# The rows of x turned by VectorE and moved through memory, in a two-layer mixture-of-experts kernel

## The chip, the cores and the metric

The kernel runs on one core of a Trainium2 chip. The metric is the device time of one execution in microseconds (us), the median of three runs. TensorE multiplies, VectorE and ScalarE work on what it leaves, GpSimd issues the indirect DMAs (rows picked by an index), SyncE the loads of weights. All DMAs run on 16 shared DMA engines.

## What is computed

```python
x = attention(q, k, v, mem_k, mem_v)              # (3072, 512) after a reshape
# layer 1: each row of x goes to its best 2 of 8 experts
logits = x @ w_gate + np.log1p(np.exp(x @ w_noise)) * noise
for e in range(8):
    for k in range(2):
        mask = top2[:, k] == e
        h = np.maximum(x[mask] @ w1[e], 0.0)      # (rows, 512) @ (512, 1024)
        out[mask] += top2_w[mask, k, None] * (h @ w2[e])
# layer 2: the same on that output, the best 1 of 8, other weights
        out[mask] = gate_w[mask, None] * (np.maximum(xe @ w1[e], 0.0) @ w2[e])
```

All in float32. The kernel keeps float32 precision by splitting each operand in a high and a low part and adding three products (high by high, high by low, low by high).

## The kernel before

A front part computes attention, gates and routing tables (to about 190 us, and a second, shorter one from about 766 to 860 us). The rest is the two expert layers, class `Experts`, instances `x` and `z`. Rows are sorted by expert and cut in tiles of 128, each with one expert: 53 tiles in the first layer, 27 in the second. What is said here of tile t holds for both.

For one tile: GpSimd copies the row numbers to `from_row` and gathers 128 rows of x (`gather`, L1552) into `xg`. TensorE turns them by four transposes of 128x128 (`x_transposes`, L1594) into PSUM `ps_x`, since a product wants the 512 inputs on the partitions. ScalarE writes the high part `x_hi` (`high_x`, L1672), VectorE the low part `x_lo` (`low_x`, L1699). `first_product` is 24 matmuls of 512 columns into `ps_h`. h is not turned by TensorE: VectorE turns it in blocks of 32x32 in two instructions (`turn`, L1710) into `h_turned`, ScalarE's queue stores that to the memory tensor `h_d` (`park`, L1658) and reads it back in four DMAs with the blocks in their places (`fetch`, L1667) into `h_moved`. There is one `h_d` and one `h_moved`: a park waits until the fetch before it has landed (semaphore `moved`), and a fetch waits until `low_h` has read the last contents (`h_split`). ScalarE makes `h_hi` (`high_h`, L1681), VectorE `h_lo` in four instructions (`low_h`, L1719). `second_product` is 24 matmuls into `ps_y`; ScalarE weighs the result by its gate into `y` (`weigh`, L1693), and GpSimd adds it to the output rows (`scatter`, L1580; in the second layer it stores them, L1583).

The order is written out by hand in one loop for each engine, and each engine works through its own in order. TensorE (`tensor_loop`), iteration t: first product t+1, transposes t+2, second product t-1. ScalarE (`scalar_loop`): high_x t+2, park t+1, high_h t, weigh t-1, fetch t+1. VectorE (`vector_loop`): some pieces of the next expert's weights (`splits`, L141 and L147, two instructions each), turn t+1, low_x t+2, more pieces, low_h t. How many pieces stand at the two places of a tile is in two tables (`before`, `middle`) that the kernel works out from the routing. GpSimd (`pool_loop`): wait for the transposes t+3, keep the gate t+3 (`keep_gate`, L1561, copies one column of `xg`), gather t+4, scatter t. Below, a tile of VectorE is called light when no pieces stand between low_x and low_h, and heavy when two do. A period is the time from one tile's transposes to the next tile's.

## Time and profile before

| | us |
|---|---|
| median of three runs | 1152.98 (1149.24 to 1154.13) |
| the profiled execution, its own time | 1158.04 |
| its span in the trace | 1156.1 |
| TensorE busy | 1094.8 |
| VectorE busy | 643.2 |
| GpSimd busy | 317.6 |
| ScalarE busy | 279.9 |

Busy time is the time in which an engine executed something; a share is of the span. The mean granted clock of TensorE in the profiled execution was 0.963 of 2.4 GHz. In a timeline, the bracket at a row's end gives how long the engine had been idle before it, and what ended the wait. A row of a queue (ACTq) is the issue of a DMA, not its transfer.

### The profile page before, as it was taken

To read this page: it belongs to the slowest core of one execution; us is meant where nothing else is said; L and a number is where in the kernel's file an instruction comes from. 1 tells how busy PE (TensorE), PEld (TensorE's weight loads), DVE (VectorE), ACT (ScalarE), POOL (GpSimd) and SP (SyncE) were. 2 spreads that over 40 slices of the span, in tenths; PEclk is the share of its full clock that TensorE was granted. 3 is DMA by queue.
4 is the path that set the end of the run, shared out by engine and by line. 5 is a ranking of instruction groups with operands and counts; after the bars stand their busy time and mean duration, and the time that the engine had idled before them with its cause. 6 is when DMAs were issued, how large, how long until landed. Compare 5 with 4: busy or idle time off the path is not lost. (4 is left out here: it accounts for less than half of the span.)

```text
span 1156.1 us, 29685 instructions
## 1 busy us (share of the span) xinstructions
PE 1094.8 (95%) x7939; PEld 886.5 (77%) x7940; DVE 643.2 (56%) x1360; ACT 279.9 (24%) x534; POOL 317.6 (27%) x474
## 2 busy tenths in 40 slices
PE   5989888999999999999999999979989999999997
PEld 4767766888888888888888888856567888877785
DVE  2767586655553552644635436306876336666862
ACT  3566321121211212121212112115212121212121
...
GB/s 344 348 344 280 294 273 148 239 221 217 183 234 143 213 209 137 227 196 165 235 175 204 219 135 211 137 96 270 61 246 241 193 124 219 247 232 236 303 222 88
DMA packets 126990, 245.87 MB, mean 213 GB/s; under 512 B 17454, under 2 KB 70878, under 8 KB 126960
## 3 DMA queue, kind: packets, MB, share of 16 engines
...
q10 hardware_dynamic: 61728, 90.25, 24.2%
...
q8 instruction: 14, 0.23, 0.1%
...
## 5 line engine op out<-in xcount | busy, mean ns | idle before, releaser
L1601 PE MATMUL moe_ps_h<-weights,moe_x_hi 128*128 (+1 forms) x640 | 253.8, 397 | 11.2 <-ACT moe_x_hi L1672 7.9
L1601 PE MATMUL moe_ps_y<-weights,moe_h_hi 128*128 (+1 forms) x624 | 251.6, 403 | 6.4 <-ACT moe_h_hi L1681 4.9
L1602 PE MATMUL moe_ps_h<-weights,moe_x_hi 128*128 (+1 forms) x640 | 251.8, 393 | 0.0
L1602 PE MATMUL moe_ps_y<-weights,moe_h_hi 128*128 (+1 forms) x624 | 244.5, 392 | 0.0
L1719 DVE SCALAR_TENSOR_TENSOR moe_h_lo<-moe_h_moved,moe_h_hi 128x256 fp32r<-128x256 f32 x312 | 111.5, 420 | 228.6 <-ACT moe_h_hi L1681 228.6
L1606 PE MATMUL moe_ps_h<-weights,moe_x_lo 128*128 (+1 forms) x640 | 172.9, 392 | 0.0
L1681 ACT ACTIVATE moe_h_hi<-moe_h_moved 128x1024 fp32r<-128x1024 f32 x78 | 82.7, 1060 | 371.0 <-PE moe_ps_y L1606 301.6
L147 DVE TENSOR_TENSOR weights<-stage,weights (+1 forms) x128 | 156.7, 1225 | 19.7 <-DVE weights L141 19.7
L1606 PE MATMUL moe_ps_y<-weights,moe_h_lo 128*128 (+1 forms) x624 | 154.1, 389 | 0.0
L1601 PEld LDWEIGHTS moe_ps_h<-weights,moe_x_hi 128*128 128x128 f32 x640 | 121.6, 190 | 41.5 <-issue 13.8
L1601 PEld LDWEIGHTS moe_ps_y<-weights,moe_h_hi 128*128 128x128 f32 x624 | 117.9, 189 | 31.5 <-issue 6.1
L1606 PEld LDWEIGHTS moe_ps_h<-weights,moe_x_lo 128*128 128x128 f32 x640 | 121.5, 190 | 25.6
L1602 PEld LDWEIGHTS moe_ps_h<-weights,moe_x_hi 128*128 128x128 f32 x640 | 121.7, 190 | 25.2 <-issue 0.2
L1672 ACT ACTIVATE moe_x_hi<-moe_ps_x 128x512 fp32r<-128x512 f32 x82 | 49.1, 599 | 374.1 <-PE moe_ps_x L1594 289.3
L1710 DVE STREAM_TRANSPOSE moe_h_turned<-moe_ps_h 128x512 f32<-128x512 f32 x160 | 107.5, 699 | 57.6 <-issue 35.7
L1606 PEld LDWEIGHTS moe_ps_y<-weights,moe_h_lo 128*128 128x128 f32 x624 | 117.1, 188 | 24.3
L1602 PEld LDWEIGHTS moe_ps_y<-weights,moe_h_hi 128*128 128x128 f32 x624 | 118.0, 189 | 22.4
L1580 POOL DMA_INDIRECT x_d<-moe_y,moe_to_row x51 | 82.7, 1621 | 187.0 <-ACT moe_y L1693 185.1
L141 DVE TENSOR_SCALAR weights<-stage (+1 forms) x124 | 85.1, 687 | 74.8 <-issue 74.7
L1552 POOL DMA_INDIRECT moe_xg<-x_d,moe_from_row x83 | 99.5, 1199 | 72.0 <-POOL moe_from_row L1546 35.4
L1561 POOL COPY routes_gate<-moe_xg (+2 forms) x81 | 17.7, 218 | 202.7 <-PE moe_ps_x L1594 194.4
L1699 DVE TENSOR_TENSOR moe_x_lo<-moe_ps_x,moe_x_hi 128x512 fp32r<-128x512 f32 x82 | 55.0, 671 | 26.0 <-ACT moe_x_hi L1672 26.0
...
## 6 DMA issues: line engine op xcount, KB each, us to landing
stage<-in_w SPq DMA_DIRECT2D x128, 512.0 KB, 4.5
...
moe_h_moved<-h_d ACTq DMA_DIRECT2D x320, 128.0 KB, 3.4
...
```

The costliest lines, as they stand in the source:

```text
L141: dve.tensor_scalar(weights[:, to, :], stage[:, frm, :], 1.0, None, ALU.mult).then_inc(sem("w_high"), 1)
L147: dve.tensor_tensor(weights[:, to + NCHUNK, :], stage[:, frm, :], weights[:, to, :].bitcast(F32), ALU.subtract).then_inc(sem("split"), 1)
L1552: pool.indirect_dma_start(xg[:, :], None, self.x_rows[0:among, :], at, bounds_check=among - 1, oob_is_err=True).then_inc(s("gathered_b" if ...
L1580: d = pool.indirect_dma_start(self.y_rows, at, y[:, :], None, bounds_check=NPAD - 1, oob_is_err=True, compute_op=ALU.add)
L1601: pe.matmul(out, a_hi, b_hi, start=(i == 0), stop=False)
L1602: pe.matmul(out, a_hi, b_lo, start=False, stop=False)
L1606: mm = pe.matmul(out, a_lo, b_hi, start=False, stop=(i == len(parts) - 1))
L1672: act.activation(self.x_hi[:, :, :], self.ps_x[:, :, :], ACT.Copy).then_inc(self.s("x_high"), 1)
L1681: act.activation((self.h_hi_end if end else self.h_hi)[:, :, :].rearrange("p c (a q) -> p c a q", a=QB), self.h_moved[:, :, :, :].rearrang ...
L1699: dve.tensor_tensor(self.x_lo[:, :, :], self.ps_x[:, :, :], self.x_hi[:, :, :].bitcast(F32), ALU.subtract)\
L1710: dve.transpose(self.h_turned[:, 2 * f:2 * f + 2, :, :].rearrange("p b c q -> p (b c q)"), self.ps_h[:, f, :]).then_inc(s("turned"), 1)
L1719: last = dve.scalar_tensor_tensor(out=h_lo[:, :, cols], in0=self.h_moved[:, a, :, :], scalar=0.0, in1=h_hi[:, :, cols].bitcast(F32), op0=A ...
```

## The change

In the loops of both layers TensorE turns no rows of x any more. From tile 5 in the first layer and tile 4 in the second, VectorE turns them in blocks of 32x32 in one instruction (`turn_x`) into a new buffer `x_turned`. ScalarE's queue stores it to a new memory tensor `xt_d` (`park_x`) and reads it back in four DMAs (`fetch_x`) into a new buffer `x_moved`, in contiguous runs of 128 numbers (h: 256). `high_x` and `low_x` read `x_moved` in SBUF instead of `ps_x` in PSUM; `high_x` then waits for the first product before it by a semaphore of its own, since no transposes stand between. The semaphores are `x_parked` and `x_moved`; `xt_done` is now counted up by turn_x. The first tiles still go over TensorE.

The order changes with it. VectorE, tile t: pieces, turn t+1, low_x t+2, **turn_x t+4**, pieces, low_h t. ScalarE: high_x t+2, park t+1, **fetch_x t+3**, high_h t, weigh t-1, fetch t+1, **park_x t+4**. GpSimd: **scatter t first**, then wait for tile t+5 to be turned, keep its gate, **gather t+6** (LAG = 5). So scatter t and gather t+6 fall in the same period, and VectorE turns that row tile in the next one. At the start of each layer one more tile is gathered ahead into a second buffer `xg_b`. The number of pieces at each place, the weight loads and all products are as before.

```diff
+LAG = 5
...
             x.gather(pool, 0)
-            for t in range(1, EARLY):
-                pool.wait_ge(s("xt_done"), t)
-                x.keep_gate(pool, t - 1)
-                x.gather(pool, t)
+            x.gather(pool, 1, second=True)
+            pool.wait_ge(s("xt_done"), 1)
+            x.keep_gate(pool, 0)
+            x.gather(pool, 2)
+            pool.wait_ge(s("xt_done"), 2)
+            x.keep_gate(pool, 1, second=True)
...
             x.scatter(pool, 0)
-            m = x.tiles(pool)
-            pool.wait_ge(s("xt_done"), EARLY + 1)
-            x.keep_gate(pool, EARLY)
-            x.gather(pool, EARLY + 1)
-            x.pool_loop(pool, 1, m)
+            m = x.gathered_ahead(pool)
+            pool.wait_ge(s("xt_done"), 4)
+            x.keep_gate(pool, 3)
+            x.gather(pool, 4)
+            x.gather(pool, 5, second=True)
+            pool.wait_ge(s("xt_done"), 5)
+            x.keep_gate(pool, 4)
+            x.gather(pool, 6)
+            pool.wait_ge(s("xt_done"), 6)
+            x.keep_gate(pool, 5, second=True)
+            pool.memset(x.xg_b[:, DM:DM + E], 0.0)
+            x.pool_loop(pool, m)
...
-        self.gathers = 16 if routes.k == 2 else 0
+        self.turned_from = 5 if routes.k == 2 else 4
+        self.xt_d = xt_d
+        self.x_blocks = xt_d.rearrange("(a p) (b r) -> b p a r", a=QB, b=QB)
...
+            self.x_turned = sb("x_turned", [P, QB, DC, QR])
+            self.x_moved = sb("x_moved", [P, QB, DC, QR])
...
+    def gathered_ahead(self, eng):
+        return self.table(eng, self.routes.full, 1, self.routes.least + 1 - LAG, self.routes.tiles + 1 - LAG)
...
+    def park_x(self, act, t):
+        s, n = self.s, t - self.turned_from
+        act.wait_ge(s("xt_done"), t + 1)
+        if not (isinstance(t, int) and n == 0):
+            act.wait_ge(s("x_moved"), n * (16 * QB))
+        act.dma_start(self.xt_d, self.x_turned[:, :, :, :].rearrange("p b c q -> p (b c q)"))\
+           .then_inc(s("x_parked"), 16)
+    def fetch_x(self, act, t):
+        s, n = self.s, t - self.turned_from
+        act.wait_ge(s("x_parked"), n * 16 + 16)
+        act.wait_ge(s("x_split"), t)
+        for b in range(QB):
+            act.dma_start(self.x_moved[b * QR:(b + 1) * QR, :, :, :].rearrange("p a c q -> p a (c q)"),
+                          self.x_blocks[b]).then_inc(s("x_moved"), 16)
+    def high_x(self, act, t, moved=False):
+        s, n = self.s, t - self.turned_from
+        if moved:
+            act.wait_ge(s("x_moved"), n * (16 * QB) + 16 * QB)
+            act.wait_ge(s("l1_done"), t * 2)
+            act.nop(nofuse=True)
+            act.activation(self.x_hi[:, :, :].rearrange("p c (a q) -> p c a q", a=QB),
+                           self.x_moved[:, :, :, :].rearrange("p a c q -> p c a q"), ACT.Copy).then_inc(s("x_high"), 1)
+        else:
+            act.wait_ge(s("xt_done"), t + 1)
+            act.activation(self.x_hi[:, :, :], self.ps_x[:, :, :], ACT.Copy).then_inc(s("x_high"), 1)
...
-    def low_x(self, dve, t):
+    def low_x(self, dve, t, moved=False):
         dve.wait_ge(self.s("x_high"), t + 1)
-        dve.tensor_tensor(self.x_lo[:, :, :], self.ps_x[:, :, :], self.x_hi[:, :, :].bitcast(F32), ALU.subtract)\
-           .then_inc(self.s("x_split"), 1)
+        if moved:
+            last = dve.tensor_tensor(self.x_lo[:, :, :].rearrange("p c (a q) -> p c a q", a=QB),
+                                     self.x_moved[:, :, :, :].rearrange("p a c q -> p c a q"),
+                                     self.x_hi[:, :, :].bitcast(F32).rearrange("p c (a q) -> p c a q", a=QB),
+                                     ALU.subtract)
+        else:
+            last = dve.tensor_tensor(self.x_lo[:, :, :], self.ps_x[:, :, :], self.x_hi[:, :, :].bitcast(F32),
+                                     ALU.subtract)
+        last.then_inc(self.s("x_split"), 1)
+    def turn_x(self, dve, t, second=False):
+        s, xg = self.s, self.xg_b if second else self.xg
+        if second:
+            dve.wait_ge(s("gathered_b"), 32)
+        else:
+            dve.wait_ge(s("gathered"), t * 16 - 16)
+            dve.wait_ge(s("x_parked"), (t - self.turned_from) * 16)
+        dve.nop(nofuse=True)
+        dve.transpose(self.x_turned[:, :, :, :].rearrange("p b c q -> p c b q"),
+                      xg[:, 0:DM].rearrange("p (c b q) -> p c b q", c=DC, b=QB)).then_inc(s("xt_done"), 1)
...
-        def tile(t, end=False):
+        def tile(t, first=False, end=False):
             frm, mid, to = self.counts(dve, t, (before, t), (middle, t), (before, t + 1))
             dve.wait_ge(s("l2_done"), t)
             dve.nop(nofuse=True)
             self.splits(dve, frm, mid)
             self.turn(dve, t + 1)
-            self.low_x(dve, t + 2)
+            if not end:
+                self.low_x(dve, t + 2, moved=not first)
+            if first:
+                self.turn_x(dve, t + 3, second=True)
+            if not first and not end:
+                self.turn_x(dve, t + 4)
             self.splits(dve, mid, to)
             self.low_h(dve, t, end)
-        with dve.Fori(begin, m) as t:
+            if first:
+                self.turn_x(dve, t + 4)
+        tile(begin, first=True)
+        with dve.Fori(begin + 1, m) as t:
             tile(t)
         tile(m, end=True)
...
     def scalar_loop(self, act, begin, m):
-        def tile(t, end=False):
-            self.high_x(act, t + 2)
+        def tile(t, first=False, end=False):
+            if not end:
+                self.high_x(act, t + 2, moved=not first)
             self.park(act, t + 1)
+            if first:
+                self.park_x(act, t + 3)
+            elif not end:
+                self.fetch_x(act, t + 3)
             self.high_h(act, t, end=end)
             if end:
                 self.fetch(act, t + 1)
...
             else:
                 self.weigh(act, t - 1)
                 self.fetch(act, t + 1)
-        with act.Fori(begin, m) as t:
+            if first:
+                self.fetch_x(act, t + 3)
+            if not end:
+                self.park_x(act, t + 4)
+        tile(begin, first=True)
+        with act.Fori(begin + 1, m) as t:
             tile(t)
         tile(m, end=True)
         self.high_h(act, m + 1, last=m)
         self.weigh(act, m, end=True)
         self.weigh(act, m + 1, last=True)
+        near = self.gathered_ahead(act)
+        act.wait_ge(self.s("x_parked"), near * 16 + (3 - begin) * 16)
+        act.wait_ge(self.s("x_moved"), near * (16 * QB) + (2 - begin) * (16 * QB))
+        act.nop(nofuse=True)
     def tensor_loop(self, pe, begin, m):
         with pe.Fori(begin, m + 1) as t:
             self.first_product(pe, t + 1)
-            self.x_transposes(pe, t + 2)
             self.second_product(pe, t - 1)
         self.second_product(pe, m, end=True)
         self.second_product(pe, m + 1, last=True)
-    def pool_loop(self, pool, begin, m):
+    def pool_loop(self, pool, m):
         s = self.s
-        with pool.Fori(begin, m) as t:
-            pool.wait_ge(s("xt_done"), t + 4)
+        with pool.Fori(1, m) as t:
+            self.scatter(pool, t)
+            pool.wait_ge(s("xt_done"), t + (LAG + 1))
             pool.nop(nofuse=True)
-            self.keep_gate(pool, t + 3)
-            self.gather(pool, t + 4)
-            self.scatter(pool, t)
-        self.scatter(pool, m, end=True)
-        self.scatter(pool, m + 1, last=True)
-        pool.wait_ge(s("gathered"), m * 16 + (48 + self.gathers))
+            self.keep_gate(pool, t + LAG)
+            self.gather(pool, t + (LAG + 1))
+        for i in range(LAG - 1):
+            self.scatter(pool, m + i, end=(i == LAG - 3), last=(i == LAG - 2))
+        pool.wait_ge(s("gathered"), m * 16 + (LAG - 1) * 16)
         if self.add:
-            pool.wait_ge(s("scattered"), m * 16 + 32)
+            pool.wait_ge(s("scattered"), m * 16 + (LAG - 1) * 16)
         else:
-            pool.wait_ge(s("scattered"), m * 16 + 16)
+            pool.wait_ge(s("scattered"), m * 16 + (LAG - 2) * 16)
             pool.wait_ge(s("scattered_last"), 16)
         pool.nop(nofuse=True)
...
+        xt_d = nc.dram_tensor("xt_d", [P, DM], F32, kind="Internal").ap()
```

VectorE, in the loop of the first layer, from the second turn of h to the wait of the pieces behind low_x. Before (`ps_h` is the first product; `staged` is the loaded piece of weights):

```order
L1710 STREAM_TRANSPOSE moe_h_turned<-moe_ps_h 128x512 [waits moe1_l1_done]
L1698 REGISTER_ALU
L1699 TENSOR_TENSOR moe_x_lo<-moe_ps_x,moe_x_hi 128x512 [waits moe1_x_high]
L1725 COMPARE_AND_BRANCH
L1726 UNCONDITIONAL_BRANCH
L1726 ISA
L141 REGISTER_ALU [waits staged]
```

With the change:

```order
L1783 STREAM_TRANSPOSE moe_h_turned<-moe_ps_h 128x512 [waits moe1_l1_done]
L1752 REGISTER_ALU
L1754 TENSOR_TENSOR moe_x_lo<-moe_x_moved,moe_x_hi 128x512 [waits moe1_x_high]
L1769 ISA
L1770 ISA [waits moe1_gathered]
L1772 STREAM_TRANSPOSE moe_x_turned<-moe_xg 128x4x4x32 [waits moe1_x_parked]
L1798 COMPARE_AND_BRANCH
L1799 UNCONDITIONAL_BRANCH
L1799 ISA
L142 REGISTER_ALU [waits staged]
```

The row with `moe_x_turned` has moved in between low_x and the pieces, with a wait for `gathered` and one for `x_parked`.

ScalarE, in the same loop, from its second step on. Before:

```order
L1655 ISA
L1657 REGISTER_ALU [waits moe1_turned]
L1658 DMA h_d<-moe_h_turned 128x1024 [waits moe1_moved]
L1679 ISA [waits moe1_l2_done]
L1681 ACTIVATE moe_h_hi<-moe_h_moved 128x1024 [waits moe1_moved]
L1693 ISA [waits moe1_gated,moe1_l2_done,moe1_y_free]
L1693 ACTIVATE moe_y<-moe_ps_y,routes_gate 128x512
L1663 ISA
L1667 DMA moe_h_moved<-h_d 32x4x256 [waits moe1_h_split,moe1_parked]
```

With the change:

```order
L1681 ISA
L1683 REGISTER_ALU [waits moe1_turned]
L1684 DMA h_d<-moe_h_turned 128x1024 [waits moe1_moved]
L1708 ISA
L1709 REGISTER_ALU [waits moe1_x_parked]
L1711 DMA moe_x_moved<-xt_d 32x4x128 [waits moe1_x_split]
L1711 DMA moe_x_moved<-xt_d 32x4x128 x3
L1732 ISA [waits moe1_l2_done]
L1734 ACTIVATE moe_h_hi<-moe_h_moved 128x1024 [waits moe1_moved]
L1746 ISA [waits moe1_gated,moe1_l2_done,moe1_y_free]
L1746 ACTIVATE moe_y<-moe_ps_y,routes_gate 128x512
```

The four DMAs `moe_x_moved<-xt_d` have moved in between the park of h and high_h; the fetch of h (L1693) and the store of x (L1702) follow.

GpSimd, in the same loop, from the loop's head. Before, it begins with the gate:

```order
L1561 ISA
L1561 COPY routes_gate<-moe_xg 128x1
L1481 ISA [waits moe1_gated]
L1481 TENSOR_LOAD routes_place
L1481 ISA x2
L1546 ISA
L1546 COPY moe_from_row<-routes_row 128x1
L1548 REGISTER_ALU
L1552 DMA moe_xg<-x_d,moe_from_row 128x520 [waits moe1_from_row]
```

With the change it begins with the scatter, and the gate's copy and the gather come behind:

```order
L1598 COPY moe_to_row<-routes_row 128x1
L1600 REGISTER_ALU
L1601 REGISTER_ALU [waits moe1_to_row]
L1605 DMA x_d<-moe_y,moe_to_row 3200x520 [waits moe1_y_ready]
L1893 REGISTER_ALU
L1503 ISA [waits moe1_xt_done]
L1503 TENSOR_LOAD routes_expert
L1503 ISA x2
L1586 ISA
L1586 COPY routes_gate<-moe_xg 128x1
```

The scatter, which waits for y, now stands ahead of the gather.

## Rows read from the trace of the kernel before

**Rows 1.** The page: busy us (share of span) and count; queue: packets, MB, share.
```profile
PE 1094.8 (95%) x7939; PEld 886.5 (77%) x7940; DVE 643.2 (56%) x1360; ACT 279.9 (24%) x534; POOL 317.6 (27%) x474
...
q10 hardware_dynamic: 61728, 90.25, 24.2%
```

**Rows 2.** Stretches: length, busy time of each engine, clock, DMA share, GB/s.
```profile
430.22:441.57 11.35, 11.35 (x54) 9.40 (x52) 3.55 (x7) 2.24 (x3) 3.26 (x5) 1.00 0.53 139
464.27:475.62 11.35, 11.35 (x54) 9.40 (x52) 8.80 (x13) 2.24 (x3) 3.67 (x5) 1.00 0.92 269
1058.00:1107.00 49.00, 46.55 (x210) 37.44 (x209) 41.84 (x60) 8.95 (x12) 20.32 (x21) 1.00 0.89 282
```

**Rows 3.** Transposes of x in each layer's loop: count, ns min/median/max, first and last start.
```profile
L1594 PE MATMUL moe_ps_x<-ident,moe_xg x192: 270/272/273, 214.6 to 748.3; 128*128 128x128 f32 x192
...
L1594 PE MATMUL moe_ps_x<-ident,moe_xg x96: 270/272/273, 862.2 to 1130.4; 128*128 128x128 f32 x96
```

**Rows 4.** Timeline of TensorE around one tile's transposes: start, duration.
```profile
407.52 0.60 PE L1594 MATMUL moe_ps_x<-ident,moe_xg 128*128 128x128 f32 x4
407.87 0.48 PE L1601 MATMUL moe_ps_y<-weights,moe_h_hi 128*128 x1
408.19 0.39 PE L1602 MATMUL moe_ps_y<-weights,moe_h_hi 128*128 x1
408.42 0.40 PE L1601 MATMUL moe_ps_y<-weights,moe_h_hi 128*128 x1
```

**Rows 5.** Timeline of ScalarE and its queue in a light tile.
```profile
427.74 1.76 ACTq L1667 DMA_DIRECT2D moe_h_moved<-h_d  x4
...
433.79 0.34 ACTq L1658 DMA_DIRECT2D h_d<-moe_h_turned  x1
436.47 1.06 ACT L1681 ACTIVATE moe_h_hi<-moe_h_moved 128x1024 fp32r<-128x1024 f32 x1 [5.01 <-PE moe_ps_y L1606]
437.43 0.67 ACT L1693 ACTIVATE moe_y<-moe_ps_y,routes_gate 128x512 f32<-128x512 f32 x1
439.07 1.76 ACTq L1667 DMA_DIRECT2D moe_h_moved<-h_d  x4
```

**Rows 6.** Timeline of GpSimd in the same tile and the next.
```profile
438.97 1.61 POOL L1580 DMA_INDIRECT x_d<-moe_y,moe_to_row  x1 [4.02 <-ACT moe_y L1693]
443.03 0.18 POOL L1561 COPY routes_gate<-moe_xg  x1 [2.46 <-PE moe_ps_x L1594]
...
445.02 1.08 POOL L1552 DMA_INDIRECT moe_xg<-x_d,moe_from_row  x1 [0.83 <-DMA x_d<-moe_y,moe_to_row]
```

**Rows 7.** Timeline of VectorE: a light tile, then a heavy one.
```profile
430.49 0.72 DVE L1710 STREAM_TRANSPOSE moe_h_turned<-moe_ps_h 128x512 f32<-128x512 f32 x1 [0.60 <-PE moe_ps_h L1606]
...
437.56 1.43 DVE L1719 SCALAR_TENSOR_TENSOR moe_h_lo<-moe_h_moved,moe_h_hi 128x256 fp32r<-128x256 f32 x4 [5.38 <-ACT moe_h_hi L1681]
...
463.49 0.69 DVE L141 TENSOR_SCALAR weights<-stage  x1 [1.80 <-issue]
464.36 1.23 DVE L147 TENSOR_TENSOR weights<-stage,weights  x1 [0.17 <-DVE weights L141]
465.50 1.30 DVE L1710 STREAM_TRANSPOSE moe_h_turned<-moe_ps_h 128x512 f32<-128x512 f32 x2
466.73 0.65 DVE L1699 TENSOR_TENSOR moe_x_lo<-moe_ps_x,moe_x_hi 128x512 fp32r<-128x512 f32 x1
467.31 0.67 DVE L141 TENSOR_SCALAR weights<-stage  x1
...
471.61 1.43 DVE L1719 SCALAR_TENSOR_TENSOR moe_h_lo<-moe_h_moved,moe_h_hi 128x256 fp32r<-128x256 f32 x4 [0.24 <-ACT moe_h_hi L1681]
```

**Rows 8.** DMA issues (KB, us to landing), and the indirect ones of both layers.
```profile
moe_h_moved<-h_d ACTq DMA_DIRECT2D x320, 128.0 KB, 3.4
...
L1552 POOL DMA_INDIRECT moe_xg<-x_d,moe_from_row x83: 1032/1080/2044, 137.0 to 1132.9; - x83
...
DMA to landing us min/median/max: 3.3/4.5/7.5
...
L1583 POOL DMA_INDIRECT out<-moe_y,moe_to_row x25: 1023/1032/2014, 860.2 to 1142.2; - x25
```

**Rows 9.** Timelines in the second layer: GpSimd beside two pieces; VectorE's low_h, consecutive heavy tiles.
```profile
1062.51 2.03 POOL L1552 DMA_INDIRECT moe_xg<-x_d,moe_from_row  x1 [0.85 <-POOL moe_from_row L1546]
...
1069.32 1.42 DVE L1719 SCALAR_TENSOR_TENSOR moe_h_lo<-moe_h_moved,moe_h_hi 128x256 fp32r<-128x256 f32 x4
...
1081.53 1.42 DVE L1719 SCALAR_TENSOR_TENSOR moe_h_lo<-moe_h_moved,moe_h_hi 128x256 fp32r<-128x256 f32 x4
```

**Rows 10.** Pieces of weights split in the loop of each layer: count.
```profile
L141 DVE TENSOR_SCALAR weights<-stage x56: 669/691/696, 236.8 to 724.6; - x56
...
L141 DVE TENSOR_SCALAR weights<-stage x48: 670/686/714, 863.5 to 1126.3; - x48
```

**Rows 11.** Timeline of TensorE: the third tile's transposes.
```profile
162.23 0.94 PE L1594 MATMUL moe_ps_x<-ident,moe_xg 128*128 128x128 f32 x4 [2.01 <-DMA moe_xg<-x_d,moe_from_row]
```

33 lines of the change are left out of this document (19 added, 14 removed).

## The prediction

> **What bounds the kernel now.** I read the summary first: TensorE 95% busy, VectorE 56%, ScalarE 24% [rows 1]. The share of an average says little, so next the table of stretches. A light tile of the first expert layer (no weights to split) takes 11.35 us, with TensorE full and the clock at 1.00, that is 2.4 GHz; so does a heavy one, with VectorE busy 8.80 us and the DMA engines at 0.92; in the second layer a run of heavy tiles has TensorE idle for 2.45 of 49 us at a DMA share of 0.89 [rows 2]. The count of transposes gives the whole: 192, four to a tile, from 214.6 to 748.3 us, so 47 periods of 11.35 us = 533.4 us in the first layer; 96 from 862.2 to 1130.4 us, so 23 periods = 267.8 us in the second (11.64 us each) [rows 3]. So TensorE bounds the first layer outright. The other engines run in step, and what they have is slack inside a period, not time to give away. The question is which slack the change uses up.
>
> **What is removed.** Transposes begin at 407.52 and the second matmul behind them at 408.19; matmuls follow each other by 0.23, so the four cost TensorE 0.67 - 0.23 = 0.44 us [rows 4]. Take 0.45: a period that TensorE bounds falls from 11.35 to 10.90 us. 73 of the 82 groups go, 49 and 24. If nothing else came late that would be 73 x 0.45 = 33 us. VectorE's subtraction reads SBUF in place of PSUM: 0.65 us before, against half of the 1.23 of one 1024 wide from SBUF, 0.62 [rows 7], so nothing.
>
> **What is added on ScalarE, and where it lies.** ScalarE's loop through h is a closed chain: fetch of h issued at 427.74, all of it landed and so h_d free and the next park issued at 433.79 (6.05 us); high_h starts at 436.47, held only by TensorE; it takes 1.06, VectorE's low_h 1.43 follows, and the next fetch is issued at 439.07, 2.60 us after high_h began [rows 5]. Without TensorE's hold this chain would take 6.05 + 0.34 + 2.60 = 9.0 us of 11.35. The change puts the four issues of the x fetch between park and high_h. Four issues of the same kind hold the queue for 1.76 us [rows 5]. Chain: 6.05 + 0.34 + 1.76 + about 0.1 to hand over + 2.60 = **10.85 us**, against the new period of 10.90. A light tile thus still fits, with nothing left; a delay, once there, is no longer made up. The store of x and its issue come behind the fetch of h, off this chain.
>
> **What is added on VectorE, and what it waits for.** One transpose of 128x512 per tile, from SBUF: 0.65 us by its sibling from PSUM (1.30 for two); bounds 0.35, half of the split's first operation of 0.69 on 1024 columns in SBUF, and 0.72, a sibling that stands alone [rows 7]. What matters is its place: behind low_x and ahead of the second splits and of low_h, and behind a wait for the gather. GpSimd now scatters a tile before it gathers the one that VectorE turns in the next tile. From high_h's end at 437.53 [rows 5]: scatter starts 1.44 later at 438.97 and takes 1.61; from the gate copy to the gather's start is 445.02 - 443.03 = 1.99 [rows 6]; between scatter and gate copy I take 0.4 (the rows allow 0, as the copy behind the gather starts at once, to 0.9, the wait of the others); issue to landing is 4.5 us, 3.3 to 7.5 [rows 8]. The row of x is there 1.44 + 1.61 + 0.4 + 1.99 + 4.5 = 9.94 us after high_h's end, and turned at 10.6. The next low_h may start at 10.9. So in a light tile the wait is covered by VectorE's idle time ahead of low_h, 5.38 us in such tiles [rows 7].
>
> In a **heavy tile** it is not covered. Before, the two splits of the second half ran from 467.31 and low_h followed at 471.61, 4.3 us later and only 0.24 of it a wait [rows 7]: they began as soon as low_x was done. Now they begin when the gather has come. 9.94 + 0.65 + 0.3 (branch and loop no longer hidden behind a queued operation; 0 to 0.5) + 4.0 = **14.9 us** from high_h's end to the next low_h, against 10.85. Behind low_h stand the fetch of h on ScalarE, hence the park, the x fetch, high_h and the weighing, and then TensorE's second product. A heavy tile delays the chain by 4.0 us.
>
> **Where the Trainium skill is weighed against the trace.** Beside VectorE's splits a gather's issue on GpSimd takes 2.03 us [rows 9], by the median 1.08 [rows 8], 0.95 more. The gather now comes 12 to 13 us after the end of a first product, where the next tile's first split may run; 14.9 + 0.95 = 15.8 us is the upper value of a heavy tile, and I take the median row since of two heavy tiles in four the split may miss it. The Trainium skill states this as a rule (SBUF — State Buffer, the box on the "DVE blocks DMA" trap: a DMA of GpSimd's queue waits for its descriptors while VectorE holds the shared port pair in a two-port operation). The skill has a rule against the change itself (VectorE: DVE Perf Modes, Rules for kernel authors): a 128x128 transpose belongs on TensorE where PSUM will do as the destination. By the rule the loss would be there in every tile; by the rows the two cost 0.44 us of one engine and 0.65 of the other, and only the waits decide.
>
> **The sum.** First layer: 56 pieces are split in the loop [rows 10], eight for each of seven experts, in four tiles as 3, 1, 3, 1, so 14 heavy tiles of the 47. 14 x 14.9 + 33 x 10.9 = 568.3; less the slack before TensorE is reached, once. high_h's results are wanted when the second product starts, 0.35 behind 441.57; the weighing ends at 438.10, so 3.8, and 3.5 with the shorter period [rows 2, 5]. 564.8 against 533.4: **+31**. Second layer: 48 pieces, four to a tile, so 12 heavy tiles [rows 10], 7 of them behind a light one. Its scatter takes 1.03 in place of 1.61 [rows 8], so 14.3 each; the 5 that follow a heavy tile are bound by VectorE itself, 12.21 from one low_h to the next [rows 9], plus 0.65 and 0.3 = 13.2; 11 light ones at 10.9. 100.1 + 66.0 + 119.9 - 3.5 = 282.5 against 267.8: **+15**. Startup: the third tile waited 2.01 us for its gather [rows 11], which is now issued a tile earlier: **-2**, or nothing if the routing tables end the wait instead. DMA: the queue of h moved 90.25 MB in 24.2% of the span, 280 us, so 3.1 us a MB [rows 1]; x's round trip is 0.52 MB a tile, 1.6 us of all engines. Its store is issued right behind the fetch of h, whose landing is in the chain. Bounds: 0, and 1.6 in each of the 44 light tiles, 70 us. I take 0.35, under half of the store's 0.8: **+15**. Together 31 + 15 - 2 + 15 = **+59**. The profiled execution took 1158.0 us (span 1156.1 and 1.9 around it), 5 above the median of 1153.0. 1217 on its scale, 1212 on the median's, of which I give **1210**.
>
> **Rivals.** The floor of all of them is 70 periods of 10.9 us, 763 against the 801.2 of before, so -38. (1) *The waits are shorter than I give them, and the kernel gains.* h's fetch lands in 5.5 us (one issue of it lands in 3.4 [rows 8], and the fourth is issued 1.4 behind the first), so a light tile makes up 0.6; the gather lands in its least of 3.3, and the 0.4 and 0.3 fall away, so a heavy tile takes 1.44 + 1.61 + 1.99 + 3.3 + 0.65 + 4.0 = 13.0, 2.1 over the period. 26 x 2.1 = 55, less 44 x 0.6 = 26 made up, less the slack of 3.5 twice: +22. With -38 and -2: 1158 - 18 = 1140, 1135 on the median's scale. With no loss at all 1118. For it: light tiles are not late by my sum either, and the losses are sums of guesses of a few tenths. Against: nothing in the order takes the second splits from behind the wait. (2) *The DMA engines become the bound.* Share 0.92 of 11.35 is 10.4 us in a heavy tile [rows 2]; with 1.6 more it is 12.0, over the period, and each landing in the chain grows. 0.5 us more in each of the 44 light tiles (+22) and 15.8 for a heavy one (26 x 0.9 = +23): 1255. (3) *A wash.* As (1), but a heavy tile 2.9 over: 26 x 2.9 = 75, less 26 and 7, less 40: +2, that is 1155. That the change doesn't do what it says is left out: the order has no transposes of x in TensorE's loops; the five and four tiles ahead of them are in the sum.
>
> **How the numbers follow.** The forecast (the chain closes at about 10.9 us and heavy tiles stretch it) 0.60; the DMA bound 0.17; the gain 0.17; the wash 0.06. The point is the forecast's, 1210. Its own range is 1175 to 1240. The wide one reaches into both outer cases and leaves out the far half of the gain and the top of the DMA case: 1130 to 1262. A measurement of this kernel tells about 0.5%, 6 us, from no change. Faster by more than that (below 1147): 0.17; within it: 0.06; slower: 0.77.
>
> **What would show it.** Right: no transposes of x on TensorE in the loops, and light tiles at 10.9 to 11.4 us; the new transpose on VectorE idle in front of it, released by the gather; in heavy tiles low_h late and TensorE waiting for high_h, for y or for the turned h, three or four us each; ScalarE's high_h released by DMA or by VectorE, no longer by TensorE. Wrong: TensorE full through the first layer with periods of 10.9 (then the chain is shorter than I add it up: the first suspect is the 6.05 us, the second the gather's place), or heavy tiles no longer than light ones, or gathers that land before low_x is done.

## The result: slower by an eighth, in the direction forecast and outside its range

| | before | with the change |
|---|---|---|
| median, us | 1153.56 (1149.24 to 1155.27) | 1300.78 (1292.16 to 1307.11) |
| ratio | | 1.124, 95% interval 1.119 to 1.130 |
| profiled execution: span, us | 1156.1 | 1296.8 |
| TensorE: busy, us; granted clock of 2.4 GHz | 1094.8; 0.963 | 1114.1; 0.941 |

The forecast was 1210 with a range up to 1262. The page of the changed kernel, the lines that answer to [rows 1], then the groups of its fifth section with idle time (count | busy us, mean ns of one | idle us before it, and what ended most of that):

```profile
PE 1114.1 (86%) x7647; PEld 872.7 (67%) x7648; DVE 695.5 (54%) x1435; ACT 281.1 (22%) x532; POOL 327.9 (25%) x475
...
q10 hardware_dynamic: 114576, 129.07, 31.8%
...
L1627 PE MATMUL moe_ps_h<-weights,moe_x_hi 128*128 (+1 forms) x640 | 271.2, 424 | 98.0 <-DVE moe_h_turned L1783 70.8
L1627 PE MATMUL moe_ps_y<-weights,moe_h_hi 128*128 (+1 forms) x624 | 252.5, 405 | 29.0 <-ACT moe_y L1746 23.0
...
L1734 ACT ACTIVATE moe_h_hi<-moe_h_moved 128x1024 fp32r<-128x1024 f32 x78 | 82.7, 1060 | 457.9 <-issue 428.9
...
L1772 DVE STREAM_TRANSPOSE moe_x_turned<-moe_xg 128x512 f32<-128x512 f32 x73 | 51.9, 712 | 203.2 <-DMA moe_xg<-x_d,moe_from_row 158.5
```

TensorE is busy for 19 us more, though it does less, and idle in front of both products: 98 us before the first product, mostly for VectorE's turn of h, 29 us before the second, mostly for ScalarE's weighing. VectorE's new transpose has 203 us of idle time ahead of it, 158 until a gather lands and 45 until the store of the x before has landed. The 429 us of `high_h` are put down to nothing: it waits on semaphores that the page can't place, so its wait is read from the timeline.

Stretches, with the columns of [rows 2]: a light tile (from one first product to the next), a heavy one (from one high_h to the next), a second product behind idle time, and 49 us of light tiles of the second layer.

```profile
577.31:588.75 11.44, 11.20 (x50) 8.96 (x49) 4.15 (x8) 2.27 (x3) 3.65 (x5) 1.00 0.70 185
430.25:447.06 16.81, 13.37 (x57) 10.07 (x55) 9.73 (x15) 2.26 (x3) 3.93 (x5) 1.00 0.80 223
449.16:456.35 7.19, 7.19 (x25) 5.81 (x26) 4.14 (x7) 0.63 (x1) 3.70 (x5) 0.76 0.77 197
1015.00:1064.00 49.00, 49.00 (x218) 40.57 (x217) 18.75 (x37) 10.71 (x14) 11.86 (x22) 1.00 0.61 194
```

From high_h to high_h the 32 light tiles of the first layer's loop take 11.8 us on average, with TensorE not full, and the 15 heavy ones 16.8. In the second layer a run of light tiles has TensorE full at 10.88 us a tile. The clock is 0.76 on average in the third stretch. TensorE's timeline there:

```profile
440.96 0.49 PE L1627 MATMUL moe_ps_h<-weights,moe_x_hi 128*128 x1 [2.86 <-DVE moe_h_turned L1783]
...
449.16 0.49 PE L1627 MATMUL moe_ps_y<-weights,moe_h_hi 128*128 x1 [2.47 <-ACT moe_y L1746]
...
450.39 0.63 PE L1627 MATMUL moe_ps_y<-weights,moe_h_hi 128*128 x1
450.82 0.63 PE L1628 MATMUL moe_ps_y<-weights,moe_h_hi 128*128 x1
...
453.37 0.39 PE L1628 MATMUL moe_ps_y<-weights,moe_h_hi 128*128 x1
453.60 0.39 PE L1627 MATMUL moe_ps_y<-weights,moe_h_hi 128*128 x1
```

TensorE was idle for 2.86 us ahead of one product and 2.47 ahead of the next, and in that one the matmuls stand 0.43 us apart for 3.4 us (1.2 GHz), in place of 0.23 (2.4 GHz). The product takes 7.19 us in place of 5.44.

**Where the time went**, by the starts of TensorE's phases in both traces. Up to the transposes of the fourth tile: 184.09 us in place of 186.74, -2.7. From there to the last second product in the first layer's loop (two more follow behind it), 663.1 in place of 561.6: +101.4. From that to the first transpose of the second layer 75.8 in place of 71.6: +4.1. From that transpose to the last second product in the second layer's loop 348.3 in place of 310.4: +37.9. Behind that the two are equal. The sum is the +140.7 between the spans. The forecast had +31 and +15 for the layers and +15 for the DMA engines.

ScalarE in a light tile, the answer to [rows 5]:

```profile
583.66 1.76 ACTq L1693 DMA_DIRECT2D moe_h_moved<-h_d  x4
585.61 0.34 ACTq L1702 DMA_DIRECT2D xt_d<-moe_x_turned  x1
586.45 0.63 ACT L1721 ACTIVATE moe_x_hi<-moe_x_moved 128x512 fp32r<-128x512 f32 x1 [3.76 <-issue]
589.67 0.34 ACTq L1684 DMA_DIRECT2D h_d<-moe_h_turned  x1
590.40 2.20 ACTq L1711 DMA_DIRECT2D moe_x_moved<-xt_d  x4
592.78 1.06 ACT L1734 ACTIVATE moe_h_hi<-moe_h_moved 128x1024 fp32r<-128x1024 f32 x1 [5.70 <-issue]
...
595.39 1.76 ACTq L1693 DMA_DIRECT2D moe_h_moved<-h_d  x4
```

From fetch to fetch: 6.01 (583.66 to 589.67) + 0.34 + 0.39 + 2.20 + 0.18 + 2.61 = **11.73 us**; forecast were 6.05 + 0.34 + 1.76 + 0.1 + 2.60 = 10.85. The next park waits for nothing but the landing.

A heavy tile: GpSimd, VectorE and ScalarE, the answers to [rows 6, 7]. The high_h ahead of the scatter began at 418.18.

```profile
420.68 1.61 POOL L1605 DMA_INDIRECT x_d<-moe_y,moe_to_row  x1 [4.62 <-ACT moe_y L1746]
...
424.29 1.49 POOL L1577 DMA_INDIRECT moe_xg<-x_d,moe_from_row  x1 [0.82 <-POOL moe_from_row L1571]
```

```profile
429.75 0.71 DVE L1772 STREAM_TRANSPOSE moe_x_turned<-moe_xg 128x512 f32<-128x512 f32 x1 [3.13 <-DMA moe_xg<-x_d,moe_from_row]
430.53 0.69 DVE L142 TENSOR_SCALAR weights<-stage  x1
...
434.53 1.42 DVE L1792 SCALAR_TENSOR_TENSOR moe_h_lo<-moe_h_moved,moe_h_hi 128x256 fp32r<-128x256 f32 x4
...
448.15 1.43 DVE L1792 SCALAR_TENSOR_TENSOR moe_h_lo<-moe_h_moved,moe_h_hi 128x256 fp32r<-128x256 f32 x4 [2.72 <-ACT moe_h_hi L1734]
```

```profile
436.04 2.04 ACTq L1693 DMA_DIRECT2D moe_h_moved<-h_d  x4
...
443.96 0.34 ACTq L1684 DMA_DIRECT2D h_d<-moe_h_turned  x1
444.73 2.15 ACTq L1711 DMA_DIRECT2D moe_x_moved<-xt_d  x4
447.06 1.06 ACT L1734 ACTIVATE moe_h_hi<-moe_h_moved 128x1024 fp32r<-128x1024 f32 x1 [7.33 <-issue]
```

The gather is issued 5.05 us after high_h's end (forecast 5.44) and lands 5.46 later (4.5), so VectorE's transpose starts 10.5 us after high_h's end. Behind it come the two pieces and low_h at 434.53, 3.2 us after its input was ready (high_h ended at 431.31). So far this is the forecast: low_h follows the last one (419.27) by 15.26 us. What was not forecast is behind it: the fetch of h issued at 436.04 lands, and frees the next park, only at 443.96, 7.92 us later in place of 6.0, and the tile behind a heavy one takes 13.6 us from low_h to low_h (434.53 to 448.15). In the first layer's loop this landing is 7.5 us on average behind the 14 heavy tiles that stand in it from the second expert's pieces on.

The longer landing behind a heavy tile was there before the change. ScalarE's queue in the kernel before, behind the heavy tile of [rows 7]:

```profile
473.12 2.00 ACTq L1667 DMA_DIRECT2D moe_h_moved<-h_d  x4
...
479.96 0.34 ACTq L1658 DMA_DIRECT2D h_d<-moe_h_turned  x1
```

That is 6.84 us, and 6.0 to 7.6 over the 14 heavy tiles. The turned h was ready at 478.20, so the park waited for the landing. It cost nothing there, since high_h waited for TensorE anyway.

### The profile page after: what moved, and what is told of

It reads as the page before. It is cut to its first block and busy times, and to the rows that moved or that the text cites. A ratio compares the mean times of both kernels' runs of the same rounds, so it can differ in the third digit from the quotient of the medians.

```text
span 1296.8 us, 30063 instructions
## 1 busy us (share of the span) xinstructions
PE 1114.1 (86%) x7647; PEld 872.7 (67%) x7648; DVE 695.5 (54%) x1435; ACT 281.1 (22%) x532; POOL 327.9 (25%) x475
## 5 line engine op out<-in xcount | busy, mean ns | idle before, releaser
L1627 PE MATMUL moe_ps_h<-weights,moe_x_hi 128*128 (+1 forms) x640 | 271.2, 424 | 98.0 <-DVE moe_h_turned L1783 70.8
L1628 PE MATMUL moe_ps_h<-weights,moe_x_hi 128*128 (+1 forms) x640 | 264.2, 413 | 0.0
L1627 PEld LDWEIGHTS moe_ps_h<-weights,moe_x_hi 128*128 128x128 f32 x640 | 128.8, 201 | 144.6 <-issue 117.0
L1632 PE MATMUL moe_ps_h<-weights,moe_x_lo 128*128 (+1 forms) x640 | 179.7, 404 | 0.0
L1627 PEld LDWEIGHTS moe_ps_y<-weights,moe_h_hi 128*128 128x128 f32 x624 | 119.4, 191 | 72.0 <-issue 46.2
L1605 POOL DMA_INDIRECT x_d<-moe_y,moe_to_row x51 | 89.6, 1757 | 291.5 <-ACT moe_y L1746 274.0
L1772 DVE STREAM_TRANSPOSE moe_x_turned<-moe_xg 128x512 f32<-128x512 f32 x73 | 51.9, 712 | 203.2 <-DMA moe_xg<-x_d,moe_from_row 158.5
L1628 PEld LDWEIGHTS moe_ps_h<-weights,moe_x_hi 128*128 128x128 f32 x640 | 129.3, 202 | 26.9 <-issue 0.2
L1632 PEld LDWEIGHTS moe_ps_h<-weights,moe_x_lo 128*128 128x128 f32 x640 | 127.2, 199 | 28.3
L1628 PEld LDWEIGHTS moe_ps_y<-weights,moe_h_hi 128*128 128x128 f32 x624 | 119.4, 191 | 23.7
L1721 ACT ACTIVATE moe_x_hi<-moe_x_moved 128x512 fp32r<-128x512 f32 x71 | 44.9, 632 | 371.1 <-issue 356.1
L1608 POOL DMA_INDIRECT out<-moe_y,moe_to_row x25 | 29.1, 1163 | 175.0 <-ACT moe_y L1746 166.5
```

The source lines that it names most:

```text
L1605: d = pool.indirect_dma_start(self.y_rows, at, y[:, :], None, bounds_check=NPAD - 1, oob_is_err=True, compute_op=ALU.add)
L1627: pe.matmul(out, a_hi, b_hi, start=(i == 0), stop=False)
L1628: pe.matmul(out, a_hi, b_lo, start=False, stop=False)
L1632: mm = pe.matmul(out, a_lo, b_hi, start=False, stop=(i == len(parts) - 1))
L1721: act.activation(self.x_hi[:, :, :].rearrange("p c (a q) -> p c a q", a=QB), self.x_moved[:, :, :, :].rearrange("p a c q -> p c a q"), ACT ...
L1772: dve.transpose(self.x_turned[:, :, :, :].rearrange("p b c q -> p c b q"), xg[:, 0:DM].rearrange("p (c b q) -> p c b q", c=DC, b=QB)).then ...
```

## The experiments

Three theories. **A**, the waits of the forecast: the late gather in front of VectorE's transpose holds the pieces and low_h, and the issues of x's fetch lengthen ScalarE's closed chain. **B**, the DMA engines: x's round trip makes every landing longer. **C**, TensorE: it is still the bound, or its slower clock behind idle time is. Times are medians. The kernel before ran again beside each group of runs, at 1156.4, 1159.6, 1156.4 and 1155.6 us, so differences of a few us between groups are not read.

Three of the runs (`e4_one_dma`, `e8_quarter`, `e11_small_loads`) move wrong or fewer numbers, and the second layer routes its rows by what the first puts out. Their first layer has the same tiles as the changed kernel, but their second has one tile more in two of them and three more in the last. ScalarE's weighings count them, in the changed kernel and with a quarter of x's bytes:

```profile
L1746 ACT ACTIVATE moe_y<-moe_ps_y,routes_gate x78: 667/671/689, 177.8 to 1292.4; 128x512 f32<-128x512 f32 x78
...
L1746 ACT ACTIVATE moe_y<-moe_ps_y,routes_gate x79: 665/671/688, 177.7 to 1296.2; 128x512 f32<-128x512 f32 x79
```

A tile of the second layer takes about 10 to 15 us there. So these three are compared by the length of the first layer too, from the fourth tile's transposes to its last second product: 679.3 us in the changed kernel, and 677.7 in `e6_transposes` below, which keeps its order and adds four transposes a tile.

### The two causes of theory A, one by one and together

Ahead of low_h no more (`e1_turn_last`):

```diff
-            if not first and not end:
-                self.turn_x(dve, t + 4)
             self.splits(dve, mid, to)
             self.low_h(dve, t, end)
-            if first:
+            if not end:
                 self.turn_x(dve, t + 4)
```

> Edit: VectorE turns the rows of x behind low_h, at the end of its tile, in place of ahead of the second pieces. Theory A (the transpose's wait for the gather holds the pieces and low_h behind it): in the changed kernel a heavy tile of layer 1 has the transpose at 429.75, 3.1 us of idle time ahead of it, and a heavy period is 16.8 to 17.6 us against 11.7 for a light one. Without it 14 heavy tiles of the first layer and about 12 of the second lose 3 us each, 26 x 3 = 78 less what ScalarE's chain keeps: 1235 (1220 to 1250). Theory B (x's round trip loads the DMA engines and lengthens the landings of h): nothing of that is taken away, at most 10 us: 1290. Theory C (TensorE's clock falls after gaps and the slower products set the time): fewer gaps, so as A, but light tiles change too.

Measured: 1230.3 us.

Out of ScalarE's chain (`e2_fetch_behind`):

```diff
             self.park(act, t + 1)
             if first:
                 self.park_x(act, t + 3)
-            elif not end:
-                self.fetch_x(act, t + 3)
             self.high_h(act, t, end=end)
...
                 self.weigh(act, t - 1)
+                if not first:
+                    self.fetch_x(act, t + 3)
                 self.fetch(act, t + 1)
```

> Edit: ScalarE issues the four fetches of x behind the weighing, in the time in which it waits for low_h, in place of between the park and high_h. Theory A (ScalarE's closed chain through h): a light tile falls from 11.7 us (6.0 landing, 0.34 park, 0.4, 2.2 issues, 0.2, 2.6) to 6.0 + 0.34 + 0.2 + 1.06 + 0.67 + 0.1 + 2.2 = 10.6, under TensorE's 10.88, so 33 x 0.85 = 28 us, and a heavy tile loses the 2.6 us too, 26 x 2.6 = 68, less a rest: 1225 (1205 to 1250). Theory B (DMA engines): same bytes, same engines, so 1300 within 10. If TensorE's clock sets the time, the gaps of heavy tiles remain and with them the slower products: 1270.

Measured: 1222.9 us. Both edits together (`e3_both`):

> Both edits: the transpose of x behind low_h, and the fetch of x behind the weighing. Theory A: heavy tiles keep only the slower landing of h behind a heavy tile (7.9 in place of 6.0 us), 26 x 1.9 = 49 less slack, light tiles are at 10.88: 763 + 30 + the rest, 1155 (1135 to 1175). Theory B: 1280 or more. Should the two gains be the same wait counted twice: 1215.

Measured: **1151.7 us**, ratio to before 0.996 (0.994 to 0.998). The gains of 70.5 and 77.9 us add up to the 149.1 of both together, so they are two causes and not one counted twice. The page and a stretch of the first layer's loop with both edits:

```profile
PE 1066.3 (93%) x7647; PEld 860.3 (75%) x7648; DVE 687.8 (60%) x1435; ACT 280.6 (24%) x532; POOL 315.0 (27%) x475
```

```profile
221.00:733.00 512.00, 511.44 (x2253) 422.44 (x2252) 293.84 (x492) 106.60 (x141) 176.98 (x235) 1.00 0.87 249
```

TensorE is full in 511.4 of 512 us at full clock, a tile at 10.88 us. Everything that the change cost in that layer's loop beyond its first tile was in these two places of the order.

The issues alone, made cheap in place of moved (`e4_one_dma`):

```diff
...
-        for b in range(QB):
-            act.dma_start(self.x_moved[b * QR:(b + 1) * QR, :, :, :].rearrange("p a c q -> p a (c q)"),
-                          self.x_blocks[b]).then_inc(s("x_moved"), 16)
+        act.dma_start(self.x_moved[:, :, :, :].rearrange("p a c q -> p (a c q)"), self.xt_d)\
+           .then_inc(s("x_moved"), 16)
...
```

The semaphore counts are changed to match.

> Edit: the fetch of x is one DMA of 128 partitions by 2 KB in place of four of 32 by 4 runs of 512 B, at its old place. The numbers land in the wrong places, so the output is not the reference's. The bytes are the same. Theory A (issue time in ScalarE's chain): 2.2 us become 0.45, a light tile 11.7 becomes 10.0 and so TensorE's 10.88, a heavy one loses 1.75: 33 x 0.85 + 26 x 1.75 = 73: 1227 (1210 to 1245), near what the fetch behind the weighing gives. Theory B in bytes: 1300. Theory B in packets (512 of them in place of 128): lower than A gives, under 1205.

Measured: 1242.1 us, 59 less, inside what A gives and not under the 1205 of packets. One tile more is in it. The first layer takes 626.4 us, 53 less than in the changed kernel, and 612.6, 67 less, with the fetch behind the weighing. The issue time is most of what the second edit brings.

### The gather's place on GpSimd

```diff
-            self.scatter(pool, t)
             pool.wait_ge(s("xt_done"), t + (LAG + 1))
             pool.nop(nofuse=True)
             self.keep_gate(pool, t + LAG)
             self.gather(pool, t + (LAG + 1))
+            self.scatter(pool, t)
```

> Edit: GpSimd waits for the turned tile, keeps its gate and gathers the next one ahead of the scatter, as the order was before the change; VectorE's transpose stays ahead of the second pieces. If the transpose in front of the pieces costs time only because the gather comes so late, this alone brings what moving the transpose behind low_h brought: 1230 to 1245. By the rows: in the changed kernel the transpose ends at 580.58 and the gather could be issued about 2 us later, 4.5 us sooner than now; but the transpose also waits until the store of the x before it has landed (issued 585.61, 4.7 us to landing, 590.3, against 591.3 now), so only about 1 us of the 3 is won in each heavy tile: 26 x 1 = 26, 1275 (1260 to 1290). The store's wait would then stand in front of the transpose in place of the gather's.

Measured: 1237.2 us, a gain of 63.6 where I expected 26. The place of the wait was right, its length wrong. From the waits (us in total, times, longest):

```profile
DVE moe_x_turned L1772 <- DMA xt_d<-moe_x_turned: 102.8, 51, 4.6
ACT moe_y L1746 <- POOLq L1596: 53.2, 54, 8.4
```

The store's landing is now waited for in front of the transpose 51 times, but 102.8 us in all in place of 203. The store lands in 4.0 us by the median, 4.7 in the changed kernel, and ahead of the pieces of a heavy tile the transpose starts 3.0 us ahead of high_h (432.73 and 435.69) in place of 0.5, so 2.5 us sooner and not 1. And the light tiles are shorter, 11.3 us in place of 11.8 on average: their fetch of h lands in 4.9 to 5.8 us in most of them, in place of 6.0. What of the new order makes it land sooner was not taken apart. I had taken both sizes from the changed kernel as it was, with its gather at its old time. The second row is new too: ScalarE's weighing waits until GpSimd has freed `y`. It comes back below.

### Is TensorE the bound?

Four transposes a tile back on TensorE, reading a constant, in the changed kernel (`e6_transposes`) and in the one with both edits (`e7_both_transposes`):

```diff
             self.first_product(pe, t + 1)
+            for cc in range(DC):
+                pe.transpose(self.ps_x[:, cc, :], self.ident[:, :], self.ident[:, :])
             self.second_product(pe, t - 1)
```

> Edit: the changed kernel with four transposes of 128x128 put back on TensorE between the two products, of a constant matrix into the unused bank; nothing reads them. Their 0.45 us a tile come to 73 x 0.45 = 33 us where TensorE sets the time. Theory A (TensorE is not the bound in the changed kernel, ScalarE's chain and the heavy tiles are): in the first layer nothing, in the seven or so light tiles of the second at 10.88 us some 0.45 each less their slack: 1300 to 1305. If TensorE still set the time: 1333.

> Edit: the kernel with both edits (transpose of x behind low_h, fetch of x behind the weighing; 1151.7 us), with the same four transposes put back on TensorE. There the products stand without a gap from 220.9 us to the end of the first layer, so the 0.45 us must come back in full in the first layer, 47 x 0.45 = 21, and in a part of the second, some 15 x 0.45 = 7: 1180 (1172 to 1185). Against the kernel before this also gives what the round trip costs once it delays nothing. If the products stand without a gap only because something else paces them: 1152 to 1160.

Measured: 1302.7 us against 1300.8, and 1176.0 against 1151.7. In the changed kernel the 33 us that the change takes off TensorE are worth nothing, since TensorE isn't what the tile waits for. In the kernel with both edits they cost 24 us (20 by the two ratios to the kernel before, which ran 3 us slower beside the second), and its tiles return to 11.35 us. This also measures the price of the round trip once it delays nothing in the loop: 1176.0 with the transposes kept, against 1159.6 of the kernel before beside it, ratio 1.013 (1.009 to 1.017), 15 us, in the start of the loops and in the second layer. That the slower products of theory C cost little is read and not tested: behind the slow one at 449.16 the period from high_h to high_h is 11.79 us, as in light tiles without one.

### The DMA engines

A quarter of x's bytes (`e8_quarter`), and a quarter of the weights' (`e11_small_loads`):

```diff
-        act.dma_start(self.xt_d, self.x_turned[:, :, :, :].rearrange("p b c q -> p (b c q)"))\
+        act.dma_start(self.xt_d[:, 0:P], self.x_turned[:, 0:1, :, :].rearrange("p b c q -> p (b c q)"))\
...
-            act.dma_start(self.x_moved[b * QR:(b + 1) * QR, :, :, :].rearrange("p a c q -> p a (c q)"),
-                          self.x_blocks[b]).then_inc(s("x_moved"), 16)
+            act.dma_start(self.x_moved[b * QR:(b + 1) * QR, 0:1, :, :].rearrange("p a c q -> p a (c q)"),
+                          self.x_blocks[0][:, 0:1, :]).then_inc(s("x_moved"), 16)
...
```

The rest of `x_moved` is filled once at each loop's start.

```diff
-        load_piece(sp, self.sem, self.stage, self.w, e + self.first, j)
+        at = e + self.first
+        sp.dma_start(self.stage[:, j % NSTAGE, 0:F // 4], self.w[bass.ds(at * (NCHUNK * P) + j * P, P), 0:F // 4])\
+          .then_inc(self.sem(f"stage_in{j % NSTAGE}"), 16)
```

> Edit: the changed kernel with a quarter of x's round trip: the store writes 64 KB in place of 256, each of the four fetches moves 16 KB in place of 64, with a quarter of the runs. The number of DMAs and of issues is as in the changed kernel. The output is not the reference's, since three quarters of x are not moved. Theory B (load on the DMA engines lengthens the landings): the landing of h behind a heavy tile falls from 7.9 towards 6.0 us, 26 x up to 1.9 = 49: 1255. Theory A (waits and issue times only): the issues stay at 2.2 us and the gather stays late: 1290 (1280 to 1300). My prediction's own term for the load was 15 us.

> Edit: the changed kernel with weight loads of a quarter of the columns from the second expert on (128 KB a piece in place of 512); the splits work on as many numbers as before. The output is not the reference's, since the rest of the weights is not loaded. In the changed kernel the fetch of h issued behind a heavy tile lands in 7.2 to 8.5 us, behind a light one in 6.0, and with a quarter of x's bytes it is the same. If the loads of weights on the same DMA engines cause it (three of them are issued in a heavy period), the heavy landing falls to about 6.0 and a heavy period from 16.8 to 15.0: 28 heavy tiles x 1.8 = 50, 1250 (1240 to 1265), and the loads' share in the start of the layer perhaps 5 more. If VectorE's work or the order of issues causes it, 1295 to 1300.

Measured: 1297.3 us (ratio to before 1.112 to 1.122, which overlaps the 1.119 to 1.130 of the change) and 1254.4. ScalarE behind a heavy tile, from the fetch of h to the park that waits for it; first with a quarter of x's bytes, then of the weights':

```profile
432.75 1.78 ACTq L1693 DMA_DIRECT2D moe_h_moved<-h_d  x4
...
440.70 0.34 ACTq L1684 DMA_DIRECT2D h_d<-moe_h_turned  x1
```

```profile
417.16 1.83 ACTq L1695 DMA_DIRECT2D moe_h_moved<-h_d  x4
...
422.71 0.34 ACTq L1686 DMA_DIRECT2D h_d<-moe_h_turned  x1
```

7.95 us and 5.55, against 7.92 in the changed kernel; in the second the heavy tiles of the first layer fall from 16.8 to 13.6 us on average. The landing behind a heavy tile is long because of the loads of weights, which start when pieces are split, and not because of x's own bytes. The loads lengthen the gather too: from its issue to VectorE's transpose it takes 4.35 us by the median in the first layer's loop with small loads, 5.43 in the changed kernel, and 5.40 with a quarter of x's bytes.

The medians understate both runs. With a quarter of x's bytes the first layer takes 667.7 us, 10 to 12 less than in the two executions with all of them, and the second 378.5 in place of 363.6 with its tile more. If that tile is taken off at 10 to 15 us, three quarters of x's bytes are worth 14 to 18 us. That is an estimate from single executions, and small beside the 147 us of the change. With small loads the first layer takes 623.2 us, 56 less, and three more tiles are in the 1254.4. So the 1250 that I expected was met by luck: a heavy tile lost 3.2 us where I had 1.8. None of these shares adds to the others, since the loads' landings cost time only because the new order left them no slack: with both edits and all loads in place TensorE is full in the first layer's loop.

### A version that beats both

In the first loop tile of each layer TensorE is idle. ScalarE's queue and TensorE there, in the changed kernel:

```profile
203.94 2.57 ACTq L1711 DMA_DIRECT2D moe_x_moved<-xt_d  x4
...
213.09 0.63 ACT L1721 ACTIVATE moe_x_hi<-moe_x_moved 128x512 fp32r<-128x512 f32 x1 [14.97 <-DMA moe_x_moved<-xt_d]
```

```profile
214.16 0.79 PE L1627 MATMUL moe_ps_h<-weights,moe_x_hi 128*128 x1 [9.84 <-ACT moe_x_hi L1721]
```

The fetch of x stands behind that of h (issued at 201.54), lands 9 us later, and TensorE has waited 9.84 us. It was put ahead of h's in the kernel with both edits (`e9_first_fetch`; the diff is against that kernel), and then the second layer was made as before (`e10_first_layer`):

```diff
                 self.weigh(act, t - 1)
-                if not first:
-                    self.fetch_x(act, t + 3)
+                self.fetch_x(act, t + 3)
                 self.fetch(act, t + 1)
-            if first:
-                self.fetch_x(act, t + 3)
```

> Edit: the kernel with both edits, and in the first tile of each layer's loop the fetch of x is issued ahead of the fetch of h too. In the kernel with both edits TensorE is idle for 9.4 us from 204.1 to 213.5 in the first layer's first loop tile, for the high part of x, whose fetch stands behind that of h and lands some 9 us later; in the second layer for 5.5 us. If the order of the two fetches on the queue sets this, x lands about 2 us sooner in each layer, and the slower product behind the gap stays: 1147 (1144 to 1150). If the store of x or the gather ahead of it set the time, or if the later fetch of h only moves the wait: 1152.

> Edit: as the run before it, but the second layer is as in the kernel before (TensorE turns x, GpSimd gathers ahead of the scatter, no round trip). From the first transpose of the second layer to the last second product the kernel with both edits takes 319.0 us, the kernel before 310.4: VectorE is full in pairs of heavy tiles there (13.3 us a tile). The same in the first layer is 13.3 us shorter than before. So 8.6 less the little that the earlier fetch brought in the second layer: 1140 (1136 to 1144), 1.4 per cent under the kernel before. If the saving of the first layer hung on what follows it, 1147.

Measured: 1146.0 us, ratio 0.990 (0.988 to 0.993), and **1137.6 us, ratio 0.983 (0.981 to 0.985)**. The change pays in the first layer alone, when moved out of the way there. The Trainium skill (VectorE: DVE Perf Modes, Rules for kernel authors) gives a 128x128 transpose to TensorE where PSUM will do as the destination. In the second layer the runs bear it out: from its first transpose to the last second product in its loop it takes 319.7 us with the round trip (`e9_first_fetch`) and 311.7 without. In the first, where TensorE is full, they speak against it: from the fourth tile's transposes to the last second product in the loop 544.2 us, and 561.6 in the kernel before.

Last, the same with the gather ahead of the scatter in place of the transpose behind low_h (`e12_gather_fetch`):

> Edit: as the run with the second layer of before, but in the first layer the transpose of x stays ahead of the second pieces and GpSimd gathers ahead of the scatter in its place. The gather ahead of the scatter alone brought 63 us, the transpose behind low_h 70, both taking the same wait from in front of the pieces; with the fetch of x behind the weighing as well the tiles of the first layer should stand at TensorE's 10.88 in either order: 1138 (1135 to 1148), the upper end if the transpose's wait for the store of x (2.8 us in three tiles out of four) still delays pieces.

Measured: **1352.2 us**, slower than everything. The waits that grew (us in total, times, longest), and one round of the loop that they form; L1590 is where GpSimd tells ScalarE that `y` is free:

```profile
ACT moe_y L1740 <- POOLq L1590: 186.5, 48, 8.2
...
DVE moe_x_turned L1766 <- DMA xt_d<-moe_x_turned: 168.3, 48, 6.5
```

```profile
487.73 0.69 ACT L1740 ACTIVATE moe_y<-moe_ps_y,routes_gate 128x512 f32<-128x512 f32 x1 [4.16 <-POOLq L1590]
487.90 1.78 ACTq L1705 DMA_DIRECT2D moe_x_moved<-xt_d  x4
...
493.75 0.34 ACTq L1696 DMA_DIRECT2D xt_d<-moe_x_turned  x1
...
503.62 0.69 ACT L1740 ACTIVATE moe_y<-moe_ps_y,routes_gate 128x512 f32<-128x512 f32 x1 [4.04 <-POOLq L1590]
```

```profile
499.84 0.71 DVE L1766 STREAM_TRANSPOSE moe_x_turned<-moe_xg 128x512 f32<-128x512 f32 x1 [3.89 <-DMA xt_d<-moe_x_turned]
```

```profile
501.42 0.18 POOL L1580 COPY routes_gate<-moe_xg  x1 [9.02 <-DVE moe_x_turned L1766]
...
503.58 2.07 POOL L1571 DMA_INDIRECT moe_xg<-x_d,moe_from_row  x1 [0.83 <-POOL moe_from_row L1565]
```

GpSimd frees `y` at the head of the scatter, now behind the gather; that waits for VectorE's transpose, and that for the store of the x before. The store stands on ScalarE's queue behind the weighing and waits until the fetch of x issued at 487.90 has landed. The weighing waits for `y`: from 487.73 to 503.62 once round, 15.9 us. With the scatter first, the transpose that GpSimd has waited for ahead of freeing `y` is that of the tile before, so the same steps have one period more. With the gather first alone the wait for `y` is there already (the 53.2 us above), but x's fetch, its landing included, is not in it. So my expectation failed in its ground: I had followed the two waits that each edit takes away, and not the semaphore that the two share. The loop is read from these rows and the order of the kernel; no run takes one of its steps out.

## The prediction, step by step

**What bounds, and the saving: right.** 0.45 us a tile came back in the run that put the transposes back, and the floor of 10.88 us a tile is reached as soon as nothing is late.

**ScalarE's chain in a light tile: the step that failed first.** "Four issues of the same kind hold the queue for 1.76 us" and "about 0.1 to hand over". The same issues of x took 2.15 us on average (46 groups from 220 to 840 us), and the hand-overs 0.39 and 0.18 in the tile shown. The landing (6.01 for 6.05) and the tail (2.61 for 2.60) were right. 10.85 became 11.7; the verdict "still fits, with nothing left" rested on a margin of 0.05 us, and the 1.76 stood without a bound. It was h's figure at h's place: behind the weighing x's four issues do take 1.85 us (47 groups, with both edits), so the longer time goes with their place between the park and high_h, and why is open. With 32 light tiles that is 0.86 x 32 = 28 us of the first layer's missing 70.

**The heavy tile: right in its mechanism, a term missing.** The gather in front of the transpose, the transpose in front of the pieces, low_h behind them: 15.26 us measured from low_h to low_h, 14.9 forecast. Missing was the landing of h behind it, with the loads of weights in the way. I had the loads in view only as a share of DMA time (0.92 in a heavy stretch [rows 2]), took 6.05 us of a light tile as the landing for all, and looked for the load where the new bytes were. The trace of the kernel before had 6.84 us behind the heavy tile that I read, and the changed one has 7.5 on average. The high_h periods of the heavy tiles are 16.8 us on average, and there are 15 of them, not 14: 15 x 1.9 + 4 for the one more = 32 us.

**Startup: wrong in sign.** The 2 us of the earlier gather were there (from the first tile's transposes to the third's 16.9 us in place of 18.9). But the first loop tile, whose x goes the new way with nothing ahead of it, then waits 9.8 us. From the fourth tile's transposes to that tile's high_h it took 32.4 us, before 22.7: 9.7 us. 28 + 32 + 10 = 70: the first layer's gap between +31 and +101. The slack of 3.5 us, taken once, was right: from the loop's last high_h to its second product it is 2.1 us in place of 5.5.

**DMA, +15 us: about right in size, and by luck.** It was a guess between 0 and 70. Three quarters of x's bytes are worth 14 to 18 us by the estimate above. As they lengthen the same tiles, they are a part of the gaps of the layers and not one more beside them. The rival that named the DMA engines as the bound (1255) was nearest in time and wrong in its cause as it was put: light tiles lose by issues and hand-overs; heavy ones do lose by longer landings, but these come with the weights.

**Second layer, +15 against +38.** For the heavy tiles behind a heavy one 13.2 us was forecast; four of them take 14.0 to 15.8 from low_h to low_h, and the fifth, at the start, 19.2: together 13 us over. The heavy ones behind a light one take 14.8 on average in place of 14.3, 4 us over for the seven. The 11 light ones take 11.4 on average in place of 10.9, 5 us over: 10.4 to 10.9 in a run of them, 11.6 to 12.5 singly behind a heavy one. That makes 22 of the 23 us; the start's part of it comes with TensorE idle for 6.1 us. How the rest divides between the landings and VectorE was not tested.
